# Expert layers of a fused attention and mixture-of-experts kernel: matmuls that change PSUM bank at every step

## The chip, the cores and the metric

The kernel runs on one core of a Trainium2 chip. A core has five engines that run at the same time, each with its own queue of instructions: TensorE (PE in the profile; the loading of weights into it is a row of its own, PEld), VectorE (DVE), ScalarE (ACT), GpSimd (POOL) and SyncE (SP), which here only issues DMAs. They wait for each other through semaphores. TensorE writes its results into PSUM, which has banks of 512 float32 per partition, and VectorE and ScalarE read them there. The metric is the device time of one execution in microseconds (us); lower is better.

## The reference

The program computes three layers, one after the other, on 9984 tokens of 256 features. Cut to what matters:

```
scores = z @ z.T / S;  attn = max(scores, 0) ** 2;  x = u * (attn @ v)       # 4 batches of 2496 tokens
# layer of experts 1: only tokens with x @ w_skip > 0, 8 experts, the best one of each token
e = argmax(x @ w_gate);  gate = softmax(x @ w_gate)[e]
x = x + gate * (max(x @ w1[e], 0) @ w2[e])                                   # w1 256x1024, w2 1024x256
# layer of experts 2: all tokens, 8 experts, the best one of each token
logits = x @ w_gate2 + modality_bias[modality_id]
out = gate2 * (max(x @ w1'[e], 0) @ w2'[e])
```

Every product has to be more exact than one pass in the fast float32 format gives it, so each operand is split in a high and a low part, and high x high, high x low and low x high are summed: three matmuls for one.

## The kernel before, in words

**Attention** (to about 739 us) works on chunks of 512 tokens, multiplies with u, works out gates, and scatters each token's row (features, gate, logits) to the place of its expert in a table in DRAM, `token_rows`.

**The expert part** is one loop, run in two phases (`ph` 0 and 1 in the code; phase one and phase two here), over experts and inside an expert over tiles of 256 tokens (`TT`), `t` counting on from expert to expert. With these inputs phase one has 23 tiles and phase two 40. For every tile TensorE does

- layer 1: 1024 hidden values from 256 features, as 8 blocks of 128 hidden values by 256 tokens. Each block sums 6 matmuls (2 halves of the features x 3 parts). Two blocks fill one of the four banks of `pO`; `layer1(p)` makes bank p with 12 matmuls,
- the transposes of the next tile, 4 matmuls (`transpose_in`, L1378),
- layer 2: back to 256 features, for two halves of 128 tokens, in the banks `pS0` and `pS1`. `layer2(p)` uses the hidden values of bank p: 2 blocks x 2 halves x 3 parts = 12 matmuls. In phase one layer 2 is 264 columns wide, since 8 more give the change of the second gate's logits.

A tile has 100 matmuls. Names in the profile: `ZH`, `ZL` hold the tile's features (high, low), `VH` and `VL` the weights of layer 1 and 2, `AH` and `AL` the hidden values (high, low).

**Other engines in a tile.** ScalarE takes bank p's relu into AH (L785, `h_high`), when `h_psum` says that the bank is finished; VectorE takes relu minus AH into AL (L1159, `h_low`) and counts `h_split`. ScalarE also splits the next tile's features (L734), keeps a copy of its rows (L739, after which SyncE may load a further tile), and, in the first tile of each expert, splits the next expert's weights in four pieces (L633): one behind bank 0's relu, one behind the kept copy, two behind bank 3's relu. GpSimd makes the weights' low parts (L466, four instructions for layer 1's weights and four for layer 2's), and only then loads the weights after those (L453, L454) and, in phase one, scatters the finished rows of the tile before to `token_rows` (L579). In phase one VectorE also picks the second layer's expert (L1109 to L1118, between the AL of banks 2 and 3) and works out the row's place (L1130 to L1140); ScalarE's exponent (L755) stands ahead of bank 3's relu. ScalarE's copy of the rows (L751) waits for the scatter before to land, and VectorE for that copy.

**Gate parts.** In phase one, at the start of every expert, TensorE makes eight more columns of layer 2's weights (`gate_columns`, L1360, in bank 2 of `pO`; `gate_parts`, L1370, in bank 3). ScalarE copies them out (`gcols_copied`), and VectorE takes their low part out of bank 3 (L1153, counted by `gpart_low`).

**What sets the order** is the code's own order on each engine; there is no scheduler. TensorE's order in one tile before: banks 0 and 1 of layer 1, the transposes, bank 2, layer 2 of bank 0, bank 3, layer 2 of banks 1, 2 and 3.

## Time and profile before

| | |
|---|---|
| median of 3 runs | 1570.85 us (1567.33 to 1571.03) |
| the profiled execution | 1574.07 us, its span 1572.3 us |
| TensorE matmul busy | 1514.6 us, 96% of the span, 13409 matmuls |
| weight loads busy | 1379.5 us, 88% |
| VectorE, ScalarE, GpSimd busy | 64%, 49%, 30% |
| layer 1 of the experts, L1430 | 18% of the chain that ended last |
| layer 2 of the experts, L1446 | 18% of that chain |
| mean granted TensorE clock | 0.988 of 2.4 GHz |

The span is the time from the first to the last instruction. The busy time of TensorE is the union of its matmuls' durations, which overlap: a single one lasts about 0.28 us, while they start about 0.12 us apart. So the pace is read from starts, not from durations. The expert part runs from 749 us to 1558 us.

### The profile page before, as it was taken

What the parts mean: (1) busy time and instruction counts of PE and PEld (TensorE: products, weight loads), DVE (VectorE), ACT (ScalarE), POOL (GpSimd) and SP (SyncE); (2) the same over time, 40 slices, a digit from 0 to 9 for tenths busy, and PEclk for the clock granted to TensorE, in tenths of its full rate; (3) what the DMA queues carried; (4) which work ended last, traced back from release to release, by engine and by line L of the source; (5) the groups of instructions that cost most, each with busy time, mean ns of one, the idle gap of its engine ahead of it and who ended that gap; (6) DMA issues with size and microseconds to landing.
All of it is one profiled execution on the core that took longest, in us unless ns stands there. A gap on an engine that the chain in (4) does not pass through costs nothing.

```text
span 1572.3 us, 38375 instructions
## 1 busy us (share of the span) xinstructions
PE 1514.6 (96%) x13409; PEld 1379.5 (88%) x13409; DVE 1013.3 (64%) x2382; ACT 776.4 (49%) x1463; POOL 466.1 (30%) x434
## 2 busy tenths in 40 slices
PE   8999999999999999998999999998999999999996
PEld 6878887788778887887988988988999999999996
DVE  7989977888788989876566666654333333333332
ACT  6677766676677767663444434443322322322321
POOL 4133412343133324222444444443211111111111
PEclk9999999999999999999999999998999999999998
DMA  5311031203002022112433333321311111111110
GB/s 114 95 42 49 27 109 33 63 31 99 27 29 62 27 82 80 30 40 92 139 126 114 127 129 126 99 79 46 101 48 41 48 54 41 48 48 41 48 48 26
DMA packets 60108, 106.41 MB, mean 68 GB/s; under 512 B 18183, under 2 KB 32018, under 8 KB 59980
## 3 DMA queue, kind: packets, MB, share of 16 engines
q1 hardware_dynamic: 41788, 46.66, 10.8%
q0 software_dynamic: 18192, 58.13, 10.8%
q8 instruction: 70, 1.15, 0.3%
q14 instruction: 58, 0.48, 0.1%
HBM read 75.35 MB, written 30.94 MB: 68 GB/s over the span
## 4 chain that ended last, share of the span: by engine, by line
PE 78%; DMA 6%; DVE 4%; issue 4%; POOL 3%; ACT 2%; POOLq 0%; DVEq 0%; SPq 0%; ACTq 0%
PE pO L1238 29%; PE pO L1430 18%; PE pS L1446 18%; PE pS L1227 8%; DMA token_rows<-xrow,dest 4%; POOL VL L466 2%; DMA raw<-in_v_dram 2%; PE pT L1378 1%; PE pT L1286 1%; DVE take L1110 1%; DMA A<-in_w2t_dram 1%; PE pO L1247 1%; DVE take L1109 1%; PE pM L1296 1%; PE pO L1360 1%
## 5 line engine op out<-in xcount | busy, mean ns | idle before, releaser
L1430 PE MATMUL pO<-ZH,VH 128*128 x2016 | 402.5, 288 | 2.3 <-issue 2.3
L1446 PE MATMUL pS<-VL,AH 128*128 128x256 f32 (+1 forms) x2016 | 370.3, 284 | 21.5 <-DVE AL L1159 21.5
L785 ACT ACTIVATE AH<-pO 128x512 fp32r<-128x512 f32 x252 | 151.0, 599 | 401.7 <-PE pO L1430 401.4
L1446 PEld LDWEIGHTS pS<-VL,AH 128*128 128x128 f32 x2016 | 311.8, 190 | 25.3 <-DVE AL L1159 25.2
L1430 PEld LDWEIGHTS pO<-ZH,VH 128*128 128x128 f32 x2016 | 328.3, 192 | 4.0 <-issue 4.0
L961 DVE TENSOR_TENSOR AL<-A,AH 128x512 fp32r<-128x512 f32 (+1 forms) x400 | 305.1, 763 | 13.7
L1238 PE MATMUL pO<-AH,VH 64*128 64x512 f32 (+1 forms) x1520 | 301.0, 386 | 3.7 <-DVE xT L870 2.3
L1238 PE MATMUL pO<-AH,VL 64*128 64x512 f32 (+1 forms) x1520 | 298.7, 383 | 0.0
L1238 PE MATMUL pO<-AL,VH 64*128 64x512 f32 (+1 forms) x1520 | 298.3, 382 | 0.0
L1159 DVE SCALAR_TENSOR_TENSOR AL<-pO,AH 128x512 fp32r<-128x512 f32 x252 | 172.7, 691 | 187.9 <-ACT AH L785 184.1
L659 ACT ACTIVATE R<-pS 128x512 f32<-128x512 f32 (+1 forms) x400 | 213.6, 587 | 157.5 <-PE pS L1227 148.4
L1430 PE MATMUL pO<-ZL,VH 128*128 x1008 | 286.0, 284 | 0.0
L1446 PE MATMUL pS<-VL,AL 128*128 128x256 f32 (+1 forms) x1008 | 284.6, 282 | 0.0
L959 DVE CAST AH<-A 128x512 fp32r<-128x512 f32 (+1 forms) x400 | 231.2, 578 | 44.6 <-ACT A L668 43.3
L668 ACT ACTIVATE A<-R 128x512 f32<-128x512 f32 (+1 forms) x400 | 228.1, 624 | 9.5 <-DVE AL L961 9.5
L1430 PEld LDWEIGHTS pO<-ZL,VH 128*128 128x128 f32 x1008 | 193.9, 192 | 0.0
L584 POOL DMA_INDIRECT out_dram<-xrow,tok_at x80 | 77.8, 973 | 382.9 <-DVE tok_at L1188 370.4
L1446 PEld LDWEIGHTS pS<-VL,AL 128*128 128x128 f32 x1008 | 190.8, 189 | 0.0
L1238 PEld LDWEIGHTS pO<-AH,VH 64*128 64x128 f32 x1520 | 147.8, 185 | 28.4 <-issue 3.4
L1238 PEld LDWEIGHTS pO<-AL,VH 64*128 64x128 f32 x1520 | 148.0, 185 | 23.2
L1238 PEld LDWEIGHTS pO<-AH,VL 64*128 64x128 f32 x1520 | 147.8, 185 | 22.3
L515 POOL TENSOR_TENSOR xT<-xT,uT 128x512 f32<-128x512 f32 x38 | 50.7, 1344 | 294.7 <-DVE xT L870 294.7
(194 smaller groups left out, 1584.4 us busy)
## 6 DMA issues: line engine op xcount, KB each, us to landing
raw<-in_w_dram POOLq DMA_DIRECT2D x22, 1024.0 KB, 7.1
xin<-token_rows SPq DMA_DIRECT2D x65, 268.0 KB
uT<-in_u_dram SPq DMA_DIRECT2D x16, 512.0 KB
A<-in_w2t_dram POOLq DMA_DIRECT2D x8, 1024.0 KB
raw<-in_v_dram SPq DMA_DIRECT2D x4, 1152.0 KB, 5.9
raw<-in_v_dram SPq DMA_DIRECT2D x4, 768.0 KB, 7.6
raw<-in_z_dram SPq DMA_DIRECT2D x8, 368.0 KB
token_rows<-pad_row SPq DMA_DIRECT2D x10, 268.0 KB
```

The source lines that it names most:

```text
L515: g_.tensor_tensor(xT[:, d, :], xT[:, d, :], uT[:, d, :], ALU.mult).then_inc(x_ready, 1)
L584: g_.indirect_dma_start(out, bass.IndirectOffsetOnAxis(tok_at[:, s_:s_ + 1], 0), x2a[:, s_, 0:D], None, bounds_check=N - 1, oob_is_err=Fal ...
L659: s_.activation(R[k % 2][:, 0:n], pS[k % 2][:, 0:n], ACT.Relu, scale=1.0 / S).then_inc(relu_done, 1)
L668: s_.activation(A[k % NA][:, 0:n], R[k % 2][:, 0:n], ACT.Square).then_inc(square_done, 1)
L785: s_.activation(hH[p], pO[:, p * 512:(p + 1) * 512], ACT.Relu).then_inc(q.h_hi, 1)
L959: v_.tensor_copy(AH[k % NBUF][:, 0:n], A[k % NA][:, 0:n]).then_inc(ah_ready, 1)
L961: v_.tensor_tensor(AL[k % NBUF][:, 0:n], A[k % NA][:, 0:n], AH[k % NBUF][:, 0:n].bitcast(F32), ALU.subtract).then_inc(al_ready, 1)
L1159: v_.scalar_tensor_tensor(out=hL[p], in0=pO[:, p * 512:(p + 1) * 512], scalar=0.0, in1=hH[p].bitcast(F32), op0=ALU.max, op1=ALU.subtract). ...
L1227: last = t_.matmul(pS[r][:, 0:n], w[rows, (2 * p + r) * P:(2 * p + r + 1) * P], x[rows, zc:zc + n], start=(m == 0), stop=(m == 2))
L1238: last = t_.matmul(pO[:, (KD * r + d) * QW:(KD * r + d) * QW + n], vv[rows, vo + k * D + d * P:vo + k * D + (d + 1) * P], a[k % NBUF][rows ...
L1430: last = t_.matmul(pO[:, p * 512 + fi * TT:p * 512 + (fi + 1) * TT], w[h][:, kd, f * P:(f + 1) * P], x[:, ds(par, 1), kd, :].rearrange("p ...
L1446: last = t_.matmul(pS[s][:, 0:width], a[p][:, fi * TT + s * P:fi * TT + (s + 1) * P], w[h][:, f, 0:width], start=(f == 0 and n == 0), stop ...
```

## The change

TensorE's loops alone are written anew. Layer 1 makes two banks at a time: `layer1(0)` does banks 0 and 1, `layer1(2)` banks 2 and 3, and inside it every weight block is used for one bank and then for the other, so that no two matmuls in a row write the same bank. Both banks of a pair are finished by its last two matmuls. In layer 2 the two halves of tokens, that is `pS0` and `pS1`, take turns in the innermost loop. `layer1(2)` stands ahead of all of layer 2, and waits for what bank 3 needs too: `h_split` of bank 3, and in phase one `gpart_low`.

```diff
--- before.py
+++ after.py
@@ -1419,18 +1419,21 @@
                             par = pe.snap(t % 2, min_val=0, max_val=1)
 
                             def layer1(p):
-                                pe.wait_ge(q.h_split, 4 * t + p + 1)
+                                pe.wait_ge(q.h_split, 4 * t + p + 2)
                                 if p == 2 and ph == 0:
                                     pe.wait_ge(gcols_copied, min(at + 2, E))
+                                    pe.wait_ge(gpart_low, at + 1)
                                 for fi in range(2):
-                                    f = 2 * p + fi
                                     n = 0
                                     for kd in range(KD):
                                         for w, x in ((w1h, XTH), (w1h, XTL), (w1l, XTH)):
-                                            last = t_.matmul(pO[:, p * 512 + fi * TT:p * 512 + (fi + 1) * TT], w[h][:, kd, f * P:(f + 1) * P],
-                                                             x[:, ds(par, 1), kd, :].rearrange("p o t -> p (o t)"), start=(n == 0), stop=(n == 3 * KD - 1))
+                                            for bank in (p, p + 1):
+                                                f = 2 * bank + fi
+                                                last = t_.matmul(pO[:, bank * 512 + fi * TT:bank * 512 + (fi + 1) * TT], w[h][:, kd, f * P:(f + 1) * P],
+                                                                 x[:, ds(par, 1), kd, :].rearrange("p o t -> p (o t)"), start=(n == 0), stop=(n == 3 * KD - 1))
+                                                if fi == 1 and n == 3 * KD - 1:
+                                                    last.then_inc(q.h_psum, 1)
                                             n += 1
-                                last.then_inc(q.h_psum, 1)
 
                             def layer2(p):
                                 pe.wait_ge(q.h_split, 4 * t + p + 5)
@@ -1441,8 +1444,8 @@
                                         pe.wait_ge(gpart_low, at + 1)
                                 for fi in range(2):
                                     f = 2 * p + fi
-                                    for s in range(SUB):
-                                        for n, (a, w) in enumerate(((hH, w2h), (hH, w2l), (hL, w2h))):
+                                    for n, (a, w) in enumerate(((hH, w2h), (hH, w2l), (hL, w2h))):
+                                        for s in range(SUB):
                                             last = t_.matmul(pS[s][:, 0:width], a[p][:, fi * TT + s * P:fi * TT + (s + 1) * P], w[h][:, f, 0:width],
                                                              start=(f == 0 and n == 0), stop=(f == F // P - 1 and n == 2), skip_group_check=True)
                                 last.then_inc(q.h_used, 1)
@@ -1454,11 +1457,9 @@
                                         part(t)
 
                             layer1(0)
-                            layer1(1)
                             transpose_in(q, t + 1)
                             layer1(2)
                             layer2(0)
-                            layer1(3)
                             layer2(1)
                             layer2(2)
                             layer2(3)
```

TensorE in a tile of phase one, around the start of `layer1(2)`. Before, from the transposes on (`x_loaded0` tells of the next tile's rows, `h_split0` of AL in phase one):

```order
L1378 MATMUL pT<-ident,xin 128x128 [waits x_loaded0]
L1378 MATMUL pT<-ident,xin 128x128 x3
L1422 REGISTER_ALU
L1430 MATMUL pO<-ZH,VH 128x256 [waits gcols_copied,h_split0]
L1430 MATMUL pO<-ZL,VH 128x256
L1430 MATMUL pO<-ZH,VH 128x256 x2
```

And now, at the same place:

```order
L1378 MATMUL pT<-ident,xin 128x128 [waits x_loaded0]
L1378 MATMUL pT<-ident,xin 128x128 x3
L1422 REGISTER_ALU
L1432 MATMUL pO<-ZH,VH 128x256 [waits gpart_low,gcols_copied,h_split0]
L1432 MATMUL pO<-ZH,VH 128x256
L1432 MATMUL pO<-ZL,VH 128x256 x2
```

The wait for `gpart_low` has come here from layer 2, and each matmul has a twin on the same features for the other bank.

TensorE in the same tile, layer 2 of bank 0 and what follows it. Before:

```order
L1446 MATMUL pS0<-VL,AH0 128x264 [waits gpart_low,y_out0,h_split0]
L1446 MATMUL pS0<-VL,AH0 128x264
L1446 MATMUL pS0<-VL,AL0 128x264
L1446 MATMUL pS1<-VL,AH0 128x264 x2
L1446 MATMUL pS1<-VL,AL0 128x264
L1446 MATMUL pS0<-VL,AH0 128x264 x2
L1446 MATMUL pS0<-VL,AL0 128x264
L1446 MATMUL pS1<-VL,AH0 128x264 x2
L1446 MATMUL pS1<-VL,AL0 128x264
L1422 REGISTER_ALU
L1430 MATMUL pO<-ZH,VH 128x256 [waits h_split0]
```

Now, the last rows of that block and the start of the next:

```order
L1449 MATMUL pS0<-VL,AH0 128x264
L1449 MATMUL pS1<-VL,AH0 128x264
L1449 MATMUL pS0<-VL,AL0 128x264
L1449 MATMUL pS1<-VL,AL0 128x264
L1439 REGISTER_ALU
L1449 MATMUL pS0<-VL,AH1 128x264 [waits h_split0]
L1449 MATMUL pS1<-VL,AH1 128x264
L1449 MATMUL pS0<-VL,AH1 128x264
```

`pS0` and `pS1` take turns, and layer 1's bank 3 no longer stands between layer 2 of bank 0 and of bank 1: it has moved ahead of both.

## Rows read from the trace of the kernel before

**Rows 1.** The page, section 2: TensorE's granted clock in 40 slices, in tenths.
```profile
PEclk9999999999999999999999999998999999999998
```

**Rows 2.** Stretches: length, busy time per engine (instructions), PEclk, DMA share, GB/s.
```profile
788.20:830.51 42.31, 38.67 (x348) 37.54 (x344) 26.84 (x85) 17.08 (x31) 18.51 (x17) 1.00 0.36 118
...
872.62:901.25 28.63, 26.26 (x245) 25.38 (x241) 18.76 (x54) 11.93 (x20) 16.52 (x15) 1.00 0.44 145
901.25:945.04 43.79, 40.20 (x347) 39.01 (x343) 27.63 (x87) 17.92 (x34) 18.41 (x17) 0.96 0.35 116
945.04:987.07 42.03, 38.69 (x348) 37.55 (x344) 26.73 (x85) 17.09 (x31) 18.50 (x17) 1.00 0.35 118
987.07:1025.94 38.87, 37.43 (x316) 36.74 (x312) 23.77 (x81) 16.92 (x29) 17.82 (x16) 1.00 0.31 102
...
1083.39:1546.42 463.03, 463.03 (x3900) 463.03 (x3901) 171.08 (x347) 139.85 (x238) 85.76 (x86) 1.00 0.16 50
```

**Rows 3.** Stretches: the three tiles of one expert of phase one.
```profile
830.51:844.63 14.12, 12.43 (x107) 12.18 (x104) 10.00 (x27) 8.22 (x13) 9.10 (x9) 1.00 0.40 133
844.63:857.83 13.20, 12.51 (x108) 12.25 (x107) 8.68 (x27) 3.71 (x7) 7.45 (x7) 1.00 0.54 184
857.83:872.62 14.79, 13.80 (x142) 13.18 (x140) 7.92 (x31) 5.27 (x11) 1.95 (x2) 1.00 0.21 66
```

**Rows 4.** Who waited for whom, phase one, weight loads: us, times, longest.
```profile
PEld pS L1446 <- DVE AL L1159: 25.2, 18, 2.9
```

**Rows 5.** The chain that ended last, one expert: start, us, what.
```profile
834.09 1.62 PE pO L1430 x12
837.28 3.71 DVE take L1110
...
852.44 6.89 DMA token_rows<-xrow,dest
863.80 1.73 PE pS L1446 x12
```

**Rows 6.** TensorE in order of time, layer 2 of one tile of phase two.
```profile
1302.90 0.28 PE L1446 MATMUL pS<-VL,AL 128*128 128x256 f32 x1
1303.02 0.40 PE L1446 MATMUL pS<-VL,AH 128*128 128x256 f32 x2
1303.26 0.28 PE L1446 MATMUL pS<-VL,AL 128*128 128x256 f32 x1
...
1308.37 0.39 PE L1446 MATMUL pS<-VL,AH 128*128 128x256 f32 x2
...
1309.05 0.40 PE L1446 MATMUL pS<-VL,AH 128*128 128x256 f32 x2
```

**Rows 7.** GpSimd in order of time, same expert as rows 5.
```profile
835.90 5.04 POOL L466 TENSOR_TENSOR VH<-raw,VH 128x512 fp32r<-128x512 f32 x4
843.28 5.07 POOL L466 TENSOR_TENSOR VL<-raw,VL 128x512 fp32r<-128x512 f32 x4 [2.33 <-ACT VL L633]
```

**Rows 8.** VectorE in order of time, first tiles of two experts.
```profile
832.64 0.29 DVE L1153 TENSOR_TENSOR VL<-pO,VL 128x32 fp32r<-128x32 f32 x2 [0.65 <-issue]
...
836.97 0.28 DVE L1109 TENSOR_SCALAR take<-xrow 128x2 f32<-128x2 f32 x1
...
842.24 0.69 DVE L1159 SCALAR_TENSOR_TENSOR AL<-pO,AH 128x512 fp32r<-128x512 f32 x1
...
905.63 0.29 DVE L1153 TENSOR_TENSOR VL<-pO,VL 128x32 fp32r<-128x32 f32 x2 [0.65 <-issue]
```

**Rows 9.** ScalarE in order of time, same expert as rows 5.
```profile
836.22 0.64 ACT L739 COPY xkeep<-xin 128x536 f32 x1
836.75 1.05 ACT L633 CAST VH<-raw 128x1024 fp32r<-128x1024 f32 x1
...
841.57 0.60 ACT L785 ACTIVATE AH<-pO 128x512 fp32r<-128x512 f32 x1
...
859.36 0.64 ACT L751 COPY xrow<-xrow 128x536 f32<-128x536 f32 x1 [4.88 <-DMA token_rows<-xrow,dest]
```

## The prediction, made before the changed kernel ran

> **What bounds the kernel now.** I read the clock and busy rows of the page first, then the stretches of the expert part, then the list of who waited for whom, then the chain that ended last, and at the end single rows of each engine inside one tile of 256 tokens. TensorE's granted clock is at nine tenths or more of 2.4 GHz from end to end [rows 1], so the clock is not what is wrong. The expert part has two phases. Phase two (40 tiles) runs at TensorE's pace: a stretch of 39 tiles, 463.03 us, is busy for 463.03 us with 3900 matmuls, at clock 1.00, which is 0.118 us per matmul and 11.8 a tile [rows 2]. Nothing that another engine does can make it shorter, only fewer nanoseconds between two matmuls. Phase one (23 tiles) is not like that: an expert of three tiles takes 42.31 or 42.03 us with 38.7 us busy, one of two tiles 28.63 [rows 2], and inside one of them the three tiles take 14.12, 13.20 and 14.79 us [rows 3]. Nearly all of the idle time has one name: layer 2 waiting for AL, the low half of the hidden activations, which VectorE writes: 25.2 us in 18 waits [rows 4]. The reader is to see two things. The change can work on two quantities, TensorE's pace (all 63 tiles) and these waits (phase one only); and they have nothing to do with each other.
>
> **Where the waits come from.** The chain through one expert [rows 5] goes from TensorE's layer 1 to a VectorE step, L1110, of 3.71 us, then to the scatter of rows (6.89 us), then to layer 2. L1110 is a tiny instruction on 128x2 elements. It takes 3.71 us because GpSimd subtracts weights from 835.90 for 5.04 us in four instructions of 1.26 us [rows 7]: L1110 starts at 837.28, inside the second of the four, and ends at 840.98 with the fourth. ScalarE's exponent waits for it, bank 3's relu (841.57) stands behind the exponent [rows 9], VectorE's AL of bank 3 comes at 842.24 + 0.69 [rows 8], and layer 2's last quarter needs that. This is the wait of the first tile (A). The waits of the second and third tile (B, C) are at layer 2's first quarter: GpSimd subtracts until 848.35 [rows 7], only then loads weights and scatters; the scatter lands at 859.3, ScalarE copies the staged rows at 859.36 [rows 9], VectorE follows, and layer 2 of tile C starts at 863.80 [rows 5].
>
> **The pace: nothing.** Before, a bank gets twelve matmuls in a row in layer 1 and three in layer 2; a tile changes banks about 21 times in 100 matmuls, afterwards 97 times. Layer 2 already shows what a change of bank is worth. The matmul of AL at 1302.90 writes pS0, the next one, at 1303.02, pS1: 0.12 us. From 1303.02 on, two steps inside one bank take 0.24 [rows 6]. If a bank written twice running cost time, the step at 1302.90 would be the short one. The pace is also not fixed by the bank: six matmuls take 0.68 us from 1308.37 on (0.113 each) in the same pattern of banks that elsewhere takes 0.120 [rows 6]. So I take 0 ns per matmul. The bounds are the two ends of these rows: all 63 x 96 = 6048 expert matmuls at 0.113 in place of a mean of 0.118 would give 30 us back; the other sign, 0.007 us for each of the 76 x 63 = 4800 new changes of bank, would take 33.
>
> **The order: work and waits.** No matmul, load, copy or transfer is added or taken away, and the engines other than TensorE keep their order. What moves is when banks are finished. In tile A, counted from its start (830.51), the block behind the transposes starts at 3.58 [rows 5], with as many matmuls ahead of it as before. It now has 24 matmuls and ends at 3.58 + 1.62 (the row of twelve) + 12 x 0.12 = 6.64; layer 2 starts there, 1.44 us later than it could before, and its last quarter at 6.64 + 36 x 0.121 = 11.0, as before. Bank 2 is finished 11 or 12 matmuls later than before, bank 3 earlier (6.64, against about 8.1).
> - ScalarE: relu of bank 2 and the kept copy move by 1.44. The kept copy, at 5.71 [rows 9], comes at 7.15, the second weight split at 7.68 to 8.73 (before 6.24 to 7.29).
> - GpSimd: its first two subtractions stay at 5.39 to 7.91, since the first split still comes early. The third needs the second split, so now waits until 8.73. It was ready in time before. GpSimd is idle from 7.91 to 8.73.
> - VectorE: L1109, at 6.46 [rows 8], comes at 7.90, and L1110 behind it near 8.1, in GpSimd's idle window. It takes 0.17 in place of 3.71, ends near 8.35, and the AL of bank 3, which started 1.26 behind its end, starts at 9.6 and ends at 10.3, before 11.0. A tile without a wait is 3.58 + 72 x 0.121 = 12.3 long, with 0.121 as my estimate for phase one's slightly wider matmuls (264 columns); tile A took 14.12, so its wait of 1.8 us is gone.
> - GpSimd's last subtraction: the splits of layer 2's weights come behind bank 3's relu, now near 9.5; GpSimd has them in hand when it ends the first four at 8.8 + 2.5 = 11.3, and ends all at 16.4 in place of 17.84. The scatter, its landing and ScalarE's copy (859.36) come 1.45 us earlier.
> - Tile B: layer 2 starts 1.44 later in the tile, VectorE's late start is covered: its wait (13.20 against 12.3) is gone.
> - Tile C: layer 2 starts 1.45 earlier than 33.29, at 31.84; it would be due at 2 x 12.3 + 6.7 = 31.3. A wait of 0.5 stays. From there the tile has 48 matmuls to go, not 60: 1.44 less. The expert ends 2.9 us earlier.
>
> Cover and its loss: the kept copy lets SyncE load the next tile. It comes 1.44 later, and its transposes follow a whole tile (12 us) later; nothing there. In phase two the AL of bank 3 is ready some 2.9 us after layer 1 ends (0.60 + 0.64 + 0.60 + 0.69 and the steps between), layer 2 wants it after 4.3: no wait, and no gain.
>
> The Trainium skill, "Perfetto Trace Analysis", section "Matmuls", asks for independent groups to rotate through banks so that one is emptied while the next is filled, which speaks against finishing two together. Here both are emptied under layer 2's or the transposes' matmuls, so by it too the sum stays. "SBUF — State Buffer", section "Who interferes with whom", says that whoever issues first holds the pair of ports shared by VectorE and GpSimd for a whole instruction. The row shows more than that, a wait through three instructions. By the page a missed window would cost under 1.26 us and no wait at all.
>
> **The new wait.** The second pair writes bank 3, where the gate parts of the expert's weights lie, so it now waits for gpart_low at 3.58, where layer 2 waited for it at 5.2 or later. VectorE makes it at 832.64 to 832.93, 2.4 us into the tile [rows 8]: free. Behind the expert of two tiles it isn't: there it ends at 905.92, 4.7 us into the tile that starts at 901.25, since VectorE stands behind the scatter's landing. With tiles starting earlier it would be about 5.9, TensorE stands 2.3 us, and everything behind (layer 1's rest, both relus, layer 2) with it. I count that expert at no gain.
>
> **Sum.** Four experts of three tiles (788, 830, 945 and the last) 4 x 2.9 = 11.6; the expert of two tiles (872.62), which loses waits of A and B, 28.63 - (2 x 12.3 + 1.3 for gate work) = 2.7; the expert at 901.25 0; the one at 987.07, 38.87 long with small waits, 1.5; the first has no waits. Together 15.8 us. The profiled execution took 1574.07 us, the median of the runs is 3.2 less. 1574.07 - 15.8 = 1558.3, so 1555 on the median's scale. One cannot tell less than about 0.3% (4.7 us) from no change.
>
> **Rivals.**
> 1. L1110 still misses GpSimd's window. For it: the window is 0.8 us wide and I place L1110 by 0.2 us; the order in which the two get served isn't regular (one L1109 passes, the next L1110 waits). Then tile A keeps 1.85, the scatter moves little, and each expert keeps only the 1.44 behind C's wait: five times about 1.4, 1563 to 1565.
> 2. The pace does fall, because alternating in every step does what one step of three doesn't show. For it only the spread from 0.113 to 0.120; against it the step at 1302.90. All the way it gives 1555 - 30 = 1525, half way 1540.
> 3. Changing banks costs time (the slower side): 0.007 us at each of 4800 changes is 33 us: 1555 + 33 = 1588. It decides from 15.8 + 4.7 = 20.5 us, that is 0.0043 us per change. Against it: changes at 0.12 like the rest, and an attention stage that alternates all the time at full granted clock [rows 1]. The Trainium skill, "TensorE: Matmul & The Clock Gate", section "A second HAM failure mode: psum-queue depth-cycling", tells of a kernel where cycling through banks made the clock fall to half again and again. By this rule phase two would show a clock below 1.00; the attention stage's clock disagrees.
>
> **Numbers.** Forecast (waits shrink, pace stays) 0.62; rival 1 0.18, two thirds of it still faster by over 0.3%; rival 2 0.12; rival 3 0.08. Faster 0.84, same 0.08, slower 0.08. Range 1538 to 1568: down to half of rival 2, up past rival 1.
>
> **What would show it.** Right: 39 tiles of phase two within 2 us of 463; L1110 under 0.5 us in most first tiles; the waits of layer 2 for AL at some 5 us in place of 25; a new wait of layer 1 for VectorE's VL (L1153) once. Wrong: AL waits unchanged (rival 1), a tile in phase two below 11.5 (rival 2) or above 12.1 us (rival 3).

## The result, and the profile after

The kernel after takes 1560.87 us (median of 5 runs, 1559.6 to 1561.94), the kernel before 1570.77 us (5 runs, 1567.33 to 1571.03): a ratio of 0.9943, 95% interval 0.9928 to 0.9957. The forecast was 1555 us, range 1538 to 1568, faster. It is faster by more than 0.3%; the gain is 9.9 us by the medians, 13.4 by the profiled executions (1574.07 against 1560.63).

The granted clock is what it was [rows 1]. First the page's PEclk line, then stretches (columns as in rows 2): three of the experts and the 39 tiles of phase two, and below them the three tiles of the expert at 829.14, which answer to rows 3.

```profile
PEclk9999999999999999999999999999999999999998
```
```profile
787.22:829.14 41.92, 39.65 (x348) 38.87 (x344) 24.07 (x85) 16.42 (x31) 18.44 (x17) 0.96 0.35 119
829.14:871.05 41.91, 39.65 (x347) 38.87 (x343) 24.17 (x85) 16.42 (x31) 18.38 (x17) 0.96 0.37 126
...
899.31:939.76 40.45, 38.18 (x347) 37.44 (x344) 24.07 (x85) 16.41 (x31) 18.42 (x17) 1.00 0.38 125
...
1070.70:1533.07 462.37, 462.31 (x3900) 462.11 (x3901) 163.97 (x347) 128.13 (x238) 85.79 (x86) 1.00 0.16 50
```
```profile
829.14:844.93 15.79, 13.53 (x107) 13.21 (x104) 9.41 (x27) 8.11 (x13) 12.44 (x11) 0.92 0.36 119
844.93:857.52 12.59, 12.59 (x107) 12.54 (x106) 6.96 (x27) 4.07 (x8) 4.01 (x5) 0.96 0.58 203
857.52:871.05 13.53, 13.53 (x141) 13.12 (x140) 7.80 (x31) 4.23 (x10) 1.94 (x2) 1.00 0.20 62
```

The reader is to see three things. Phase two takes 462.37 us in place of 463.03 [rows 2]. The experts of three tiles at 787.22 and 829.14 take 41.92 and 41.91, which is hardly less than 42.31 and the 42.11 that the three tiles of rows 3 add up to, though the second and third tile are shorter (12.59 and 13.53 against 13.20 and 14.79 [rows 3]). And the first tile is longer, 15.79 against 14.12, and its clock is 0.92 where it was 1.00. The large gains are elsewhere: 43.79 to 40.45 in the expert that follows the one of two tiles.

The waits of layer 2 for AL (as in rows 4) are fewer, and the ones that are left are long:

```profile
PEld pS L1449 <- DVE AL L1159: 15.4, 8, 2.5
```

15.4 us in 8 waits in place of 25.2 in 18 [rows 4]. Five of the eight are at layer 2's last quarter in a first tile, where the next matmul starts 2.55 us behind the one ahead of it, from start to start (0.12 of that is the usual step); two more there are of 1.2 us. Before, the same place had 1.97 to 2.19 us in four of the seven first tiles, and 3.00, 2.58 and 0.85 in the others. Behind two of the five the granted clock is at half (1.2 GHz): the 0.92 above. Before, it was so behind the waits of 3.00 and 2.58, in the experts at 901.25 (0.96 [rows 2]) and 1025.94.

The chain through a first tile (rows 5's place), then VectorE and GpSimd there (rows 7 and 8):

```profile
837.84 1.24 DVE eq L1115
...
841.47 0.69 DVE AL L1159
...
842.20 2.79 PE pS L1449 x12
```
```profile
837.14 0.17 DVE L1110 TENSOR_SCALAR take<-take 128x2 f32<-128x2 f32 x1
...
837.84 1.23 DVE L1115 TENSOR_TENSOR eq<-eq,rev 128x16 f32<-128x16 f32 x1
839.11 0.17 DVE L1116 TENSOR_REDUCE pick<-eq 128x2 f32<-128x16 f32 x1
839.31 1.00 DVE L1117 TENSOR_TENSOR eq<-eq,pick 128x16 f32<-128x16 f32 x1
840.35 1.19 DVE L1118 TENSOR_TENSOR oh<-eq,take 128x16 bf16<-128x16 f32 x1
841.47 0.68 DVE L1159 SCALAR_TENSOR_TENSOR AL<-pO,AH 128x512 fp32r<-128x512 f32 x1
```
```profile
834.51 2.56 POOL L466 TENSOR_TENSOR VH<-raw,VH 128x512 fp32r<-128x512 f32 x2
837.75 2.54 POOL L466 TENSOR_TENSOR VH<-raw,VH 128x512 fp32r<-128x512 f32 x2 [0.68 <-ACT VH L633]
840.24 4.98 POOL L466 TENSOR_TENSOR VL<-raw,VL 128x512 fp32r<-128x512 f32 x4
...
848.84 1.04 POOL L579 DMA_INDIRECT token_rows<-xrow,dest  x1 [1.18 <-DVE dest L1140]
```

L1110 did what was forecast: it starts at 837.14, in GpSimd's pause (837.07 to 837.75), and takes 0.17 us in place of 3.71 [rows 5]. But four steps behind it GpSimd is at work again, and L1115, L1117 and L1118 take 1.23, 1.00 and 1.19 us. Those are the steps that read two small tensors of SBUF and meet GpSimd; the reduction between them (L1116) takes 0.17, and the earlier ones with two inputs (L1113, L1114) were through by then. AL of bank 3 starts at 841.47, 12.3 us into the tile, where it started 11.7 us into it before (842.24 [rows 8]). In the chain, from L1115 to AL and layer 2's last twelve matmuls, nothing else is long.

ScalarE, as in rows 9, and VectorE in the first tile of the expert behind the one of two tiles:

```profile
835.99 0.63 ACT L739 COPY xkeep<-xin 128x536 f32 x1
836.52 1.05 ACT L633 CAST VH<-raw 128x1024 fp32r<-128x1024 f32 x1
...
855.37 0.64 ACT L751 COPY xrow<-xrow 128x536 f32<-128x536 f32 x1 [0.89 <-DMA token_rows<-xrow,dest]
```
```profile
901.41 0.29 DVE L1153 TENSOR_TENSOR VL<-pO,VL 128x32 fp32r<-128x32 f32 x2 [0.65 <-issue]
```

The kept copy of the rows comes at 6.9 us into the tile and the second weight split at 7.4 (5.71 and 6.24 before [rows 9]), as forecast (7.15 and 7.68). The scatter is in hand for ScalarE at 855.37, 26.2 us into the expert and not 28.85 [rows 9]. VL is made 2.1 us into the tile, not 4.4 [rows 8], so layer 1's second pair doesn't wait for it there. Before, VectorE stood there behind ScalarE's copy of the rows, which waits until the scatter of the expert before has landed; after, that copy is done in time. It starts 0.3 us into the expert before, and 2.1 us ahead of the expert after:

```profile
901.51 0.64 ACT L751 COPY xrow<-xrow 128x536 f32<-128x536 f32 x1 [4.98 <-DMA token_rows<-xrow,dest]
```
```profile
897.20 0.64 ACT L751 COPY xrow<-xrow 128x536 f32<-128x536 f32 x1 [2.29 <-DMA token_rows<-xrow,dest]
```

### The profile page after: what moved, and what is told of

Read it like the earlier page. It is cut to its first block, busy times and chain, and to the rows that moved or that the text cites. A ratio compares the mean times of both kernels' runs of the same rounds, so it can differ in the third digit from the quotient of the medians.

```text
span 1558.8 us, 38249 instructions
## 1 busy us (share of the span) xinstructions
PE 1509.1 (97%) x13409; PEld 1374.6 (88%) x13409; DVE 989.9 (64%) x2382; ACT 758.6 (49%) x1463; POOL 465.5 (30%) x434
## 4 chain that ended last, share of the span: by engine, by line
PE 87%; DMA 4%; DVE 3%; issue 3%; ACT 1%; POOL 1%; SPq 0%; DVEq 0%; POOLq 0%; ACTq 0%
PE pO L1238 30%; PE pO L1432 22%; PE pS L1449 21%; PE pS L1227 8%; PE pT L1378 2%; DMA raw<-in_v_dram 2%; PE pT L1286 1%; DMA A<-in_w2t_dram 1%; PE pO L1247 1%; PE pM L1296 1%; PE pO L1360 1%; DMA token_rows<-xrow,dest 1%; DMA xin<-token_rows 0%; POOL VL L503 0%; DVE eq L1115 0%
## 5 line engine op out<-in xcount | busy, mean ns | idle before, releaser
L785 ACT ACTIVATE AH<-pO 128x512 fp32r<-128x512 f32 x252 | 145.0, 598 | 466.4 <-PE pO L1432 466.3
L1432 PE MATMUL pO<-ZH,VH 128*128 x2016 | 352.8, 287 | 2.2 <-DVE ZL L1096 1.7
L1449 PE MATMUL pS<-VL,AH 128*128 128x256 f32 (+1 forms) x2016 | 323.9, 283 | 13.8 <-DVE AL L1159 13.8
L1159 DVE SCALAR_TENSOR_TENSOR AL<-pO,AH 128x512 fp32r<-128x512 f32 x252 | 169.0, 689 | 202.0 <-ACT AH L785 201.7
L1432 PEld LDWEIGHTS pO<-ZH,VH 128*128 128x128 f32 x2016 | 286.8, 192 | 4.2 <-issue 4.2
L1449 PEld LDWEIGHTS pS<-VL,AH 128*128 128x128 f32 x2016 | 276.4, 189 | 15.4 <-DVE AL L1159 15.4
L1432 PE MATMUL pO<-ZL,VH 128*128 x1008 | 203.7, 284 | 0.0
L1449 PE MATMUL pS<-VL,AL 128*128 128x256 f32 (+1 forms) x1008 | 202.7, 282 | 0.0
L1432 PEld LDWEIGHTS pO<-ZL,VH 128*128 128x128 f32 x1008 | 157.7, 192 | 0.0
L1449 PEld LDWEIGHTS pS<-VL,AL 128*128 128x128 f32 x1008 | 155.3, 189 | 0.0
```

The costliest lines, as they stand in the source:

```text
L785: s_.activation(hH[p], pO[:, p * 512:(p + 1) * 512], ACT.Relu).then_inc(q.h_hi, 1)
L1159: v_.scalar_tensor_tensor(out=hL[p], in0=pO[:, p * 512:(p + 1) * 512], scalar=0.0, in1=hH[p].bitcast(F32), op0=ALU.max, op1=ALU.subtract). ...
L1432: last = t_.matmul(pO[:, bank * 512 + fi * TT:bank * 512 + (fi + 1) * TT], w[h][:, kd, f * P:(f + 1) * P], x[:, ds(par, 1), kd, :].rearran ...
L1449: last = t_.matmul(pS[s][:, 0:width], a[p][:, fi * TT + s * P:fi * TT + (s + 1) * P], w[h][:, f, 0:width], start=(f == 0 and n == 0), stop ...
```

## Experiments

Each is compared with the kernel before by its ratio (95% interval). The edits are cut to what differs.

**1. Alternation alone, in layer 2.** The kernel before, with layer 2's inner loops exchanged, so that it changes bank at every matmul as the kernel after does.

```diff
-                                    for s in range(SUB):
-                                        for n, (a, w) in enumerate(((hH, w2h), (hH, w2l), (hL, w2h))):
+                                    for n, (a, w) in enumerate(((hH, w2h), (hH, w2l), (hL, w2h))):
+                                        for s in range(SUB):
```

> The kernel before with layer 2's two halves of tokens taking turns (pS0, pS1), and nothing else: 47 changes of bank in layer 2 of a tile where there were 16, TensorE's order of blocks as before. My theory, that the pace has nothing to do with the banks and the gain is all from the order of the blocks: 1570.8 us within 3, a tile of phase two at 11.83 to 11.85 us, and 25 us of waits of layer 2 for AL as before. The rival, that alternation gives the gain, a part of it in layer 2: about 5 us faster, with tiles of phase two below 11.75.

1569.3 us, ratio 0.9997 (0.9986 to 1.0009). The 38 tiles of phase two behind its first one, in before, in this kernel and in after:

```profile
1096.76:1546.42 449.66, 449.66 (x3802) 449.66 (x3801) 167.62 (x342) 132.59 (x228) 78.57 (x81) 1.00 0.16 51
```
```profile
1090.98:1540.64 449.66, 449.66 (x3803) 449.66 (x3801) 167.61 (x342) 132.25 (x228) 78.51 (x81) 1.00 0.16 51
```
```profile
1082.65:1533.07 450.42, 450.37 (x3802) 450.16 (x3801) 160.51 (x342) 121.17 (x228) 79.91 (x82) 1.00 0.16 50
```

449.66 and 449.66 us: changing the bank at every matmul of layer 2 neither costs nor saves anything. In after it is 450.42, 0.02 us more a tile, 0.2 ns a matmul. The waits for AL stay (24.9 us in 19).

**2. The order of after, without the alternation.** Layer 1 in two pairs, but bank by bank inside a pair, and layer 2's inner loops as before. Against after, layer 1's part:

```diff
-                                for fi in range(2):
-                                    n = 0
-                                    ...
-                                            for bank in (p, p + 1):
+                                for bank in (p, p + 1):
+                                    for fi in range(2):
+                                        n = 0
```

> The changed kernel's order of blocks (both pairs of layer 1, then all of layer 2, with its waits), but each bank filled by its twelve matmuls in a row and layer 2 in the old inner order: no alternation. If the order alone makes the gain: as fast as the changed kernel or a little faster, 1554 to 1561 us, no waits at layer 2's first quarter in phase one. Bank 2 is finished 1.4 us earlier than with alternation, so in an expert's first tile L1110 should fall on GpSimd's subtractions again and take 3 to 4 us, with a wait of 1.85 us at layer 2's last quarter in place of the 2.43 of the changed kernel: 7 x 0.6 = 4 us less. If alternation makes the gain: 1570 us.

1561.97 us, ratio 0.9944 (0.9928 to 0.996): the whole gain. One expert of it, VectorE and GpSimd (the tile starts at 826.44), and the waits:

```profile
833.17 3.69 DVE L1110 TENSOR_SCALAR take<-take 128x2 f32<-128x2 f32 x1
```
```profile
831.78 5.05 POOL L466 TENSOR_TENSOR VH<-raw,VH 128x512 fp32r<-128x512 f32 x4
```
```profile
PEld pS L1448 <- DVE AL L1159: 16.6, 11, 2.6
```

Here bank 2 ends twelve matmuls earlier than in after, GpSimd's four subtractions run without a pause, and L1110 stands behind them, 3.69 us, as before the change. A first tile keeps its wait of 1.9 us by start to start, a third tile one of 0.5 to 0.65; the waits at second tiles are gone. This is rival 1 of the prediction, whole, and it is as fast as after. What the alternation does is that the first bank of each pair ends later, bank 2 by 1.44 us.

**3 and 4. Is it the picking of the experts (L1103 to L1118) ahead of AL of bank 3?** `pick_expert` moved behind h_low(3), and ScalarE's exponent with it, in after and in before.

```diff
-                                    pick_expert(t)
                             h_low(3)
+                                    pick_expert(t)
```

> The changed kernel with VectorE's choice of the second expert (L1109 to L1118) behind the AL of bank 3, not ahead of it, and ScalarE's exponent behind bank 3's relu and one weight split. If the wait of 2.43 us in the first tile of seven experts is VectorE's two-input steps standing behind GpSimd ahead of bank 3's AL, it goes: 7 x 2.43 = 17 us and up to 3 x 1.2 us of lower clock behind it, 1540 to 1545 us. The rival, that the scatter's landing then holds the third tile: half of it comes back, 1550.

> The same move of the choice and the exponent in the kernel before, whose order of blocks stays. First tile waits (13.7 us over seven experts) go, the waits at layer 2's first quarter (10.7 us) stay, since they hang on the scatter's landing: about 1556 us. If the two edits were the same gain told twice, it would equal the run with both, near 1543; if the waits only move to the next tile, 1566 or more.

1567.87 us (0.9982, 0.9969 to 0.9996) and 1572.44 us (1.0012, 1.0 to 1.0023). Both theories missed, for a reason that the waits show:

```profile
PEld pM L1401 <- DVE oh L1116: 20.7, 8, 3.2
```
```profile
PEld pM L1401 <- DVE oh L1116: 19.6, 8, 3.2
...
PEld pS L1444 <- DVE AL L1157: 1.9, 2, 1.2
```

Layer 2 no longer waits (1.9 us are left in before), but the tile's last matmuls, the prefix of `oh`, need the picking's result, and it now comes after the tile's matmuls. The other part is the clock behind these waits: in the variant of after four of seven second tiles ran at a mean granted clock of 0.79 to 0.88 and took 1.5 to 2.8 us more than 12.17. The picking can't be put late; it is needed in the same tile.

**5. Is it GpSimd's work beside it?** In after, GpSimd's third to eighth subtraction in a first tile wait until AL of bank 3 is made.

```diff
+                    if hold is not None and n == 1:
+                        wait(PH[0].h_split, hold)
```

> The changed kernel; GpSimd does its third to eighth subtraction of each expert's weights only when the AL of bank 3 of the expert's first tile is done. If VectorE's two-input steps (L1115, L1117, L1118: 1.23, 1.00, 1.19 us in place of 0.17) are slow because GpSimd subtracts beside them, all three are back at 0.17 here and the first tile's wait at layer 2's last quarter is gone. The price is a later end of GpSimd's work by about 1.9 us, so that the scatter lands later and the third tile waits about 2 us: 1555 to 1561 us in all, about as the changed kernel. The rival, that these steps are slow for another reason (their place in the order, the exponent beside them): they stay slow, and the first tile waits 2.4 us as before.

1569.48 us, ratio 0.9996 (0.9979 to 1.0012). VectorE in a first tile (lines are two further down in this kernel), and GpSimd:

```profile
838.86 0.18 DVE L1117 TENSOR_TENSOR eq<-eq,rev 128x16 f32<-128x16 f32 x1
...
839.49 0.18 DVE L1120 TENSOR_TENSOR oh<-eq,take 128x16 bf16<-128x16 f32 x1
839.59 0.69 DVE L1161 SCALAR_TENSOR_TENSOR AL<-pO,AH 128x512 fp32r<-128x512 f32 x1
```
```profile
840.46 2.54 POOL L468 TENSOR_TENSOR VH<-raw,VH 128x512 fp32r<-128x512 f32 x2 [2.36 <-ACT VL L635]
```
```profile
PEld pS L1451 <- DVE AL L1161: 13.8, 7, 2.8
```

The three steps take 0.17 or 0.18 us in place of 1.23, 1.00 and 1.19, AL of bank 3 is early, and five of the first tiles take 12.2 us without a wait. So the subtractions beside them are the cause. The time is not the 1555 to 1561 that were expected. GpSimd starts its third subtraction 1.7 us later in the tile (10.3 and not 8.6), scatters later, and third tiles wait 1.6 to 2.8 us at layer 2's first quarter, about as expected. What was not expected: in the expert behind the one of two tiles (at 896.68) layer 1's second pair waits 4.1 us for `gpart_low`, which the 13.8 us of waits above don't hold, and the clock falls in two tiles (0.90).

**6 and 7. The picking early.** `pick_expert` ahead of h_low(0), in after and in before.

```diff
+                                    pick_expert(t)
                             h_low(0)
                             ...
-                                    pick_expert(t)
```

> The changed kernel with VectorE's choice of the second expert ahead of the AL of bank 0, in a stretch where VectorE idles for 1.3 us and GpSimd subtracts nothing; ScalarE's and TensorE's order stay. Neither the AL of bank 3 nor TensorE's prefix at the tile's end can then stand behind GpSimd. All steps of the choice at 0.2 us, no wait in the first tiles: 7 x 2.43 = 17 us and the lower clock behind some of them, 1540 to 1546 us. The rival, that the scatter's landing takes over in the third tile: 1550 to 1555.

> The same move of the choice in the kernel before. The first tiles' waits (13.7 us) go here too, but the choice's 1.8 us now stand ahead of the AL of bank 0, for which layer 2's first quarter waits in the second and third tiles already (10.7 us): these grow by up to 1.8 each, 11 tiles, so 1565 to 1575 us, no clear gain. If the changed order's 1.44 us of slack ahead of layer 2 isn't what covers this, the gain is the same as with the changed order, about 1553.

1563.22 us (0.9962, 0.9947 to 0.9976) and 1600.4 us (1.019, 1.0165 to 1.0214). Five of the seven first tiles of the first kernel take 12.18 us without a wait, but most second and third tiles get waits of 0.5 to 2.3 us:

```profile
PEld pS L1449 <- DVE AL L1159: 17.8, 14, 2.4
```
```profile
PEld pS L1446 <- DVE AL L1159: 43.5, 22, 6.7
```

In before the same move costs 30 us, where 1565 to 1575 us were expected. There AL of bank 0 is needed right behind layer 1's third bank, in after 1.44 us later; four of the first tiles wait 1.3 us for it in before's variant, and five don't wait in after's. This slack doesn't explain the two longest waits of before's variant, 6.5 and 6.7 us by start to start. VectorE and GpSimd in the first tile at 788.85 show what these are:

```profile
793.32 5.88 DVE L1117 TENSOR_TENSOR eq<-eq,pick 128x16 f32<-128x16 f32 x1
```
```profile
794.23 4.93 POOL L466 TENSOR_TENSOR VH<-raw,VH 128x512 fp32r<-128x512 f32 x4
```

One small step of the picking begins 0.9 us ahead of four subtractions and ends with the last of them. In the first tile at 1042.90 it is L1118, 5.46 us.

**8. What sets the pace.** After, with layer 1 of phase two on 128 of the 256 tokens: half the columns per matmul, as many matmuls and weight loads. It leaves half of that layer's work out.

```diff
+                                                wide = P if ph else TT
-                                                last = t_.matmul(pO[:, bank * 512 + fi * TT:bank * 512 + (fi + 1) * TT], w[h][:, kd, f * P:(f + 1) * P],
-                                                                 x[:, ds(par, 1), kd, :].rearrange("p o t -> p (o t)"), start=(n == 0), stop=(n == 3 * KD - 1))
+                                                last = t_.matmul(pO[:, bank * 512 + fi * TT:bank * 512 + fi * TT + wide], w[h][:, kd, f * P:(f + 1) * P],
+                                                                 x[:, ds(par, 1), kd, 0:wide].rearrange("p o t -> p (o t)"), start=(n == 0), stop=(n == 3 * KD - 1))
```

> The changed kernel, but in phase two layer 1 multiplies only 128 of a tile's 256 tokens: half the columns per matmul, the same weight loads of 128 columns (the other half of the hidden values is stale). If the weight loads set the pace of 0.12 us, which would explain why the bank is of no account: the step from one layer 1 matmul to the next stays above 0.105 us, the tile at 11.2 to 11.8 us. If the matmuls' own columns set it, the step falls to about 0.06 us, the tile to 9 us and the time by 110 us.

1548.53 us (one run). TensorE in order of time, layer 1 in this kernel and in after:

```profile
1125.00 0.61 PE L1433 MATMUL pO<-ZH,VH 128*128 x4
1125.45 0.39 PE L1433 MATMUL pO<-ZL,VH 128*128 x2
```
```profile
1311.77 0.64 PE L1432 MATMUL pO<-ZH,VH 128*128 x4
1312.25 0.40 PE L1432 MATMUL pO<-ZL,VH 128*128 x2
```

Four matmuls in 0.45 us against four in 0.48: 0.112 in place of 0.120 each, with half the columns. Something that comes once per matmul, whatever its columns, sets nearly all of the pace; each has its own weight load of 128 columns, and those start as far apart. No order of banks changes their number. Whether it is the load or the matmul's own start that sets it, this run doesn't separate.

**9 to 11. The picking early where there is room.** Ahead of h_low(0) in an expert's first tile alone (9), between h_low(0) and h_low(1) in every tile (10), there in first tiles alone (11). The edit of 9:

```diff
+                            if ph == 0 and at > 0:
+                                with dve.If(t == lo):
+                                    with dve.If(t > 0):
+                                        pick_expert(t)
                             h_low(0)
                             ...
-                                with dve.If(t > 0):
+                                with dve.If(t > lo):
                                     pick_expert(t)
```

> The kernel after with pick_expert ahead of h_low(0) in an expert's first tile alone; in its other tiles the picking stays behind h_low(2). Theory (the waits of layer 2's last quarter in first tiles, 6 x 2.43 + 2 x 1.2 = 17 us, come from the two-input steps L1115 to L1118 that stand behind GpSimd's subtractions; in first tiles there is time ahead of h_low(0), in the others there is none, which is why moving it in every tile brought new waits of 1.4 to 2.3 us): first tiles at 12.2 us, second and third as in the kernel after, no wait or at most 0.5 us; 1543 to 1550 us. Rival (the scatter chain takes over: with the first tile 2.4 us shorter, its landing at the tile behind ends last): waits of 1 to 2 us in each expert's third tile, 1551 to 1558 us.

> The kernel after with pick_expert between h_low(0) and h_low(1) in every tile. In a first tile VectorE is idle there (833.52 to 834.26 us in the expert that starts at 829.1) and GpSimd issues descriptors until 834.51 and subtracts only then, so theory: the picking costs a first tile under 3 us of VectorE's time, hL of bank 1 is there by 837 us, long ahead of layer 2 (about 840), first tiles at 12.2 us. In second and third tiles GpSimd subtracts or issues without a pause, so hL of bank 1 is late at layer 2's second quarter by up to 1 us: about 10 tiles x 0.5 to 1. Sum 1546 to 1556 us. Rival (what counts is only how much of the picking stands ahead of layer 2's first quarter, as in the kernel with it ahead of h_low(0)): waits of 1.4 to 2.3 us in second and third tiles again, 1558 to 1564 us.

> The kernel after with pick_expert between h_low(0) and h_low(1) in an expert's first tile alone, behind h_low(2) in the others. Theory as for the kernel with it ahead of h_low(0) in first tiles: first tiles at 12.2 us with no wait, the rest as after; 1543 to 1550 us, and within 2 us of that kernel. Rival (scatter chain, as there): 1551 to 1558 us.

9: 1556.47 us (0.992, 0.9907 to 0.9932). 10: 1565.89 us (0.9973, 0.9961 to 0.9985). 11: 1561.92 us (0.9961, 0.9947 to 0.9976). In 9 five of seven first tiles take 12.2 us without a wait, the other two wait 3.1 and 3.2 us at layer 2's first quarter (the one at 889.56 also 2.6 us for `gpart_low`), and the rival is right too: third tiles wait 1.0 to 1.5 us. In 10 and 11 the theory fell. VectorE of 11 in a first tile, and GpSimd:

```profile
832.83 2.94 DVE L1113 TENSOR_TENSOR lsh<-lg,mx 128x16 f32<-128x16 f32 x1
```
```profile
833.17 2.56 POOL L466 TENSOR_TENSOR VH<-raw,VH 128x512 fp32r<-128x512 f32 x2
```

I had counted on VectorE being through before GpSimd subtracts. L1113, which reads two tensors of SBUF, starts 0.34 us ahead of GpSimd's pair of subtractions by the records and ends 2.94 us later, with it. hL of bank 1 is late, and first tiles wait 2.96 us at layer 2's second quarter.

**12. The scatter first.** 9, and GpSimd issues the scatter of a first tile ahead of the two weight loads (in phase one).

```diff
-                            next_weights(turn_, at % 2)
+                            split_low(turn_ + 1, 1 - at % 2)
                             ...
+                            with pool.If(t == lo):
+                                load_behind(turn_)
```

> The kernel with the picking ahead of h_low(0) in first tiles, and in phase one GpSimd issues the scatter of an expert's first tile ahead of the two loads of the next weights (L453, L454), which it issued from 841.12 to 842.80 before a scatter whose rows had been placed at 841.32. Theory (the waits of 1.0 to 1.5 us in third tiles, and most of the 3.2 us at two places, are the landing of that scatter, which ScalarE's copy of the staged rows waits for): the scatter is issued near 841.6 in place of 843.10, lands 1.5 us earlier, and the waits of third tiles shrink to 0 to 0.3 us; five or six experts x 1.2 us, 1549 to 1553 us. The loads come 2.3 us later, with most of an expert to go before they are split: no wait from them. Rival (the landing is set by the traffic it shares, not by its issue): waits stay at 1.0 to 1.5 us, 1555 to 1558 us.

1550.98 us (1549.26 to 1553.55), ratio 0.9876 (0.9855 to 0.9897), the fastest kernel that does all the work. Waits of 9, then of 12; GpSimd of 12 with the scatter of one first tile's rows; VectorE of 12 in two first tiles (its lines are seven further down: L1116 is L1109 of after, L1122 and L1125 its L1115 and L1118):

```profile
PEld pS L1453 <- DVE AL L1159: 11.0, 6, 3.2
```
```profile
PEld pS L1460 <- DVE AL L1166: 5.6, 2, 3.0
```
```profile
843.48 1.01 POOL L582 DMA_INDIRECT token_rows<-xrow,dest  x1 [1.87 <-DVE dest L1147]
...
845.76 0.78 POOL L453 DMA_DIRECT2D raw<-in_w_dram  x1
```
```profile
892.40 0.38 DVE L1116 TENSOR_SCALAR take<-xrow 128x2 f32<-128x2 f32 x1 [0.67 <-issue]
...
894.15 3.31 DVE L1125 TENSOR_TENSOR oh<-eq,take 128x16 bf16<-128x16 f32 x1
```
```profile
1010.84 0.26 DVE L1116 TENSOR_SCALAR take<-xrow 128x2 f32<-128x2 f32 x1 [0.65 <-issue]
...
1011.84 3.13 DVE L1122 TENSOR_TENSOR eq<-eq,rev 128x16 f32<-128x16 f32 x1
```

The scatter goes out as soon as VectorE has placed the rows, the loads behind it. The waits of third tiles are gone, and the one of 2.6 us for `gpart_low`. The earlier issue is the smaller part of it: in this expert the scatter's second half is issued 19.3 us in and not 20.3, but ScalarE's copy of the rows, which waits for the landing, starts at 23.6 and not at 27.4. From that issue to the copy it is 4.3 us in place of 7.1, now that the two loads stand behind the scatter. So the forecast time came out, but more through what the rival names, the traffic beside the scatter, than through the earlier issue. Two waits for AL are left, 5.6 us in all, in first tiles of two experts (at 889.36 and 1006.6), and the last four lines show what they are: there the picking begins 3.0 and 4.2 us into the tile, where four of the other five first tiles have it at 2.6 (the fifth has it at 3.1, and none of its steps is slow), and its last or fourth-last step meets GpSimd and takes 3.31 and 3.13 us.

## Why the prediction was right, and where not

- **Pace nothing.** Right. 0.2 ns a matmul more, where I bounded it by -5 and +7. Experiment 1 shows it for the alternation, and experiment 8 shows why an order of banks has nothing to take hold of.
- **Waits of second and third tiles gone.** Right, and for the reason given: layer 2 starts 1.44 us later inside the tile, and has 12 matmuls fewer behind it. Experiment 2, where only this happens, has the 0.5 us at third tiles that I had worked out, and the wait for `gpart_low` (2.2 us in the tile at 894.48, forecast 2.3).
- **First tile's wait gone.** This step failed. "It takes 0.17 in place of 3.71" held; "the AL of bank 3, which started 1.26 behind its end" didn't. That term was 4.2 us (837.31 to 841.47). So that AL started 12.3 us into the tile and not at 9.6, and the waits of layer 2 for AL are 15.4 us, where I had said some 5. I took the steps behind L1110 at the length that they had before, where they ran after GpSimd had ended. GpSimd's pause moved L1110 out of its way and the two-input steps into it. The weight splits behind bank 3's relu also came early enough for GpSimd to go on without a pause, which I had written down for the scatter and not carried to VectorE. Experiment 5 shows the cause by taking it away. (The expectations count seven waits of 2.43 us in experiments 2, 3 and 6, and six in 9; there are five, and two of 1.2.)
- **The scatter earlier.** Right in sign, 1.45 us forecast, 2.6 measured (28.85 to 26.2 us into the expert). Of the 2.6 the issue is 0.9 (its second half at 21.0 us into the expert, before 21.9); the rest is a shorter way to the landing, which I had left as it was. So no wait was left at third tiles, which I had at 0.5.
- **The new wait at the expert behind the one of two tiles.** Wrong: I counted that expert at no gain, and it gained 3.3 us. VectorE no longer stood behind the scatter's landing there; the earlier scatter, which I had worked out, frees it. I used it for one place and not for this one. But only about 1.6 of the 3.3 are waits; 1.7 are that the clock, which fell behind the wait of 3.00 us before, stayed at 1.00. The wait of layer 1 for VL came once, as I had said, but in the last expert and of 0.8 us.
- **Sum.** By experts, in order:

| expert, start before | forecast, us | measured, us |
|---|---|---|
| 749.18 | 0 | 0.7 |
| 788.20 | 2.9 | 0.4 |
| 830.51 | 2.9 | 0.2 |
| 872.62 | 2.7 | 0.4 |
| 901.25 | 0 | 3.3 |
| 945.04 | 2.9 | 1.6 |
| 987.07 | 1.5 | 0.9 |
| 1025.94, with the passage to phase two | 2.9 | 4.9 |
| sum | 15.8 | 12.4 |

The sum is nearer than its terms, and that is luck: 1.3 to 2.7 us of the forecast gain are missing in each of four experts, through the failed step, and two places that I undervalued paid more than half of it back. The clock, which I had left out of the sum, moved between the lines: it fell in the experts at 901.25 and 1025.94 before, and at 787.22 and 829.14 after, 1.5 to 1.7 us each time. With that taken out, the lines of 788.20 and 830.51 would be 2.0 and 1.8, and that of 901.25 1.6. The last line is 1.9 us in its first two tiles, of which the clock is 1.5, and 3.0 in its last tile with the passage to phase two. Of these 1.2 are the third tile's wait, and 1.9 the gap ahead of phase two's first matmul (15.4 us before, 13.5 after). That gap is no gain of the change: it is 13.6 in experiment 1, whose waits are those of before, and 15.2 in experiment 2, whose order is that of after.

- **Scale.** I took 3.2 us off for the median, since the profiled execution of before was that much above it. That of after was 0.2 below its own. So 15.8 us turned into 9.9: 2.4 of the miss are the sum, 3.5 this. The 3.2 was a property of one execution, not of the program.
- **Rival 1** named the right danger (steps that stand behind GpSimd) and priced it at 1563 to 1565; experiment 2, which is that case, gave 1562, and after, in which another step stands there, 1561. **Rivals 2 and 3** are refuted by experiment 1 for layer 2, and for both layers by phase two of after (450.42 us against 449.66). Phase two's clock is 1.00 in before, after and experiment 1. The Trainium skill ("TensorE: Matmul & The Clock Gate", "A second HAM failure mode: psum-queue depth-cycling") tells of a kernel that cycles through banks, idles briefly between its groups of matmuls and has its clock swing; in phase two, which has no such idling, that doesn't show. In first tiles the clock did fall, after waits of 2.5 us.
- **Two rows read a little late.** The block behind the transposes starts 3.33 us into the tile and not 3.58 (the piece of the chain in rows 5 begins where the transposes end, and the matmuls overlap with these), and in after its 24 matmuls take 2.95 us from the first start to layer 2's, where 1.62 + 1.44 were taken. So layer 2 starts at 6.3 us and its last quarter is due at 10.6, for which I had 6.64 and 11.0; ScalarE's steps came 0.3 us earlier than forecast for it. The failed step is far larger than this.

What was needed for the failed step was at hand. The Trainium skill, "SBUF — State Buffer", "Who interferes with whom", states that a VectorE instruction with two SBUF inputs contends with a GpSimd instruction that reads SBUF, and that a reduction never does. The traces agree: L1115, L1117 and L1118 at 1.0 to 1.2 us beside GpSimd and 0.17 without it, L1116 0.17 in both. I had quoted another sentence of that section, about L1110, and not asked it of the eight steps behind.

## What to carry to other kernels

When a stall on an engine goes away, put every instruction behind it back on the clock beside what the other engine does at the new time; the stall tends to move to the next instruction that meets the same neighbour. An order of matmuls is worth what it does to the times at which others get their inputs, not what it does to the banks; here the gain came from layer 2 starting 12 matmuls later inside the tile, which covered VectorE's late start. Small steps that many wait for belong where their neighbour pauses, and not in the last microsecond before its next long row of work, and a scatter that someone waits for goes ahead of a load that nobody needs yet: those two edits gave as much again as the change itself.

## What the hardware showed that I had not expected

- A VectorE step of 0.17 us beside GpSimd's subtractions takes as long as what is left of one, or of up to four. The slow two-input steps that began inside a subtraction ended with that same one (0.9 to 1.2 us, in before, after and experiments 2, 5 and 9 to 12).
- The two-input steps that took 2.9 to 5.9 us all began 0.3 to 0.9 us ahead of a row of subtractions, while GpSimd was issuing a DMA (L458 or L579), and ended with the second or the fourth of the row: L1113 in experiment 11 (2.94), L1125 in 12 (3.31), L1117 and L1118 in 7 (5.88 and 5.46). Others that began during such an issue took 0.17. With GpSimd idle ahead of the row none was caught, as L1115 at 835.89 in experiment 11, 0.54 us ahead (0.18). I can't say from these traces which step is caught.
- L1110, with one input, is one of the slow ones when four subtractions run without a pause (3.69 us in experiment 2, from inside the second to the end of the fourth); the steps that read PSUM for one input (AL, 0.69 us) aren't.
- Halving the columns of a matmul from 256 to 128 made it 0.112 us in place of 0.120.
- A wait of 2.5 us in a stream that is otherwise full was followed by matmuls at half clock in two of five first tiles; each of the two, with the tile behind it, took 28.4 us where two others took 26.9. Before, it was so behind the two longest waits, 3.00 and 2.58 us, and not behind those of 1.97 to 2.19; in experiment 5 also behind one of 2.2, so the length of the wait alone doesn't tell.
